# Input loads of a retention, mixer and MLP kernel: the second to fourth loads each wait for an earlier landing

## The reference

```python
# retention, per head h (8 heads of 64), token by token
state = gamma[h] * state + outer(k[t], v[t]);  x[t] = scale * q[t] @ state
# token mixer with angles
theta = x @ w_theta;  zr = x * cos(theta);  zi = x * sin(theta)
u = x + w_tok_r @ zr + w_tok_i @ zi
x2 = u + relu(u @ w_ch)
# token MLP, then channel MLP
u2 = x2 + (relu(x2.T @ w_tok1) @ w_tok2).T
out = u2 + relu(u2 @ w_ch1) @ w_ch2
```

## Time and profile before

| what | value |
|---|---|
| median of 3 runs | 435.96 us (435.9 to 437.29) |
| the profiled execution's own time | 435.77 us |
| its span in the trace | 434.0 us |
| TensorE busy | 426.8 us, 98% of the span |
| VectorE, ScalarE, GpSimd busy | 278.4, 158.3, 85.3 us |
| transfers, mean over the span | 97 GB/s |
| granted TensorE clock | 9 tenths or more in all 40 slices of the page |

### The profile page before, as it was taken

The page is one execution under the profiler, slowest core; times in us unless marked ns, Lnnn a source line. Parts: engine busy times, 40 slices in busy tenths (PEclk is TensorE's granted clock), DMA queues, the critical chain, the costliest instruction groups (busy, mean ns, idle before and its releaser), DMA issues.

```text
span 434.0 us, 6621 instructions
## 1 busy us (share of the span) xinstructions
PE 426.8 (98%) x2748; PEld 388.3 (89%) x2748; DVE 278.4 (64%) x383; ACT 158.3 (36%) x231; POOL 85.3 (20%) x75
## 2 busy tenths in 40 slices
PE   7999999999999999999999999999999999999997
PEld 4778878899999999999889988888888899999997
DVE  3799998799999995234415304525211599999951
ACT  1364564744455456112214311101202443555500
POOL 1322241000300006980005803303000110000000
PEclk9999999999999999999999999999999999999999
DMA  8975797540594102030000000003000468340121
GB/s 301 419 269 198 253 270 146 103 145 2 157 220 159 48 2 97 2 115 31 0 2 0 2 0 0 2 0 142 5 0 2 72 154 171 113 67 26 54 74 73
DMA packets 10478, 42.25 MB, mean 97 GB/s; under 512 B 1104, under 2 KB 3280, under 8 KB 8656
## 3 DMA queue, kind: packets, MB, share of 16 engines
q1 hardware_dynamic: 7344, 26.74, 16.6%
q0 software_dynamic: 2960, 14.94, 15.6%
q10 hardware_dynamic: 144, 0.14, 0.1%
HBM read 38.68 MB, written 3.15 MB: 96 GB/s over the span
## 4 chain that ended last, share of the span: by engine, by line
PE 96%; DVE 2%; DMA 1%; ACT 0%; issue 0%; ACTq 0%; DVEq 0%
PE ps L982 85%; PE ps L999 3%; PE ps L1039 3%; PE ps L1053 2%; PE ps L1130 1%; PE ps L1013 1%; PE ps L1029 1%; DMA qkv_in<-qkv 1%; DVE prob L712 1%; DVE h_ops_c L906 0%; DVE w_sq L696 0%; ACT h_ops_c L657 0%; DVE x_lo L736 0%; DVE res L731 0%; DVE res L942 0%
## 5 line engine op out<-in xcount | busy, mean ns | idle before, releaser
L982 PE MATMUL ps<-u,ch 128*128 128x512 f32 x432 | 98.1, 389 | 0.0
L982 PEld LDWEIGHTS ps<-u,ch 128*128 128x128 f32 x432 | 81.1, 188 | 16.8
L982 PE MATMUL ps<-tw,zs 128*128 128x384 f32 x504 | 88.1, 335 | 0.0
L982 PEld LDWEIGHTS ps<-tw,zs 128*128 128x128 f32 x504 | 87.3, 188 | 0.1
L982 PE MATMUL ps<-h_ops_c,w 128*128 128x384 f32 x312 | 57.0, 335 | 0.2
L982 PEld LDWEIGHTS ps<-h_ops_c,w 128*128 128x128 f32 x312 | 54.2, 188 | 0.8 <-DVE h_ops_c L906 0.8
L899 DVE SCALAR_TENSOR_TENSOR h_a<-ps,h_a 128x512 f32<-128x512 f32 (+1 forms) x16 | 8.9, 558 | 44.3 <-PE ps L982 26.3
L580 ACT ACTIVATE zs<-z 128x768 fp32r<-128x768 f32 x28 | 23.7, 846 | 37.0 <-PE ps L982 37.0
L982 PE MATMUL ps<-ut,w_sq 128*128 128x384 f32 x192 | 35.5, 338 | 0.0
L982 PEld LDWEIGHTS ps<-ut,w_sq 128*128 128x128 f32 x192 | 33.0, 188 | 0.0
L982 PE MATMUL ps<-w_sq,x_hi 128*128 128x512 f32 x96 | 30.7, 401 | 0.7 <-DVE w_sq L696 0.7
(11 more groups left out here) (106 smaller groups left out, 639.0 us busy)
## 6 DMA issues: line engine op xcount, KB each, us to landing
qkv_in<-qkv SPq DMA_DIRECT2D x11, 1024.0 KB, 7.5
raw<-tok POOLq DMA_DIRECT2D x7, 1152.0 KB, 9.0
stage<-weights SPq DMA_DIRECT2D x11, 512.0 KB, 3.4
w_raw<-ch POOLq DMA_DIRECT2D x7, 768.0 KB, 6.8
cols_out<-res SPq DMA_DIRECT2D x16, 192.0 KB, 1.8
raw<-tok SPq DMA_DIRECT2D x6, 384.0 KB, 8.6
w_raw<-ch SPq DMA_DIRECT2D x2, 768.0 KB, 5.3
raw<-tok POOLq DMA_DIRECT2D x3, 384.0 KB, 9.2
```

The source lines that it names most:

```text
L982: mm = pe.matmul(dst, left(l), right(r), start=first and n == 0, stop=last and n == 2, skip_group_check=True)
```

## The change

Four waits are put into SyncE's order of loads. The second chunk is issued when the first queries and keys have landed. The two halves of the angle weights are issued when the first group's second half has landed. The third chunk is issued when the second has landed. The first third of the token weights is issued when the second half of the angle weights has landed, and what follows it on SyncE (the fourth chunk and the rest) comes behind that wait. The order of the loads is the same, and no other engine's instructions differ.

```diff
             sp.dma_start(cst[:, C_OUT:N_CONST], consts[:, C_OUT:N_CONST]).then_inc(decay_in, 16)
+
+            sp.wait_ge(first_qk_in, 16)
             load_chunk(1)
+            sp.wait_ge(chunk_in[0], 16)
             for i in range(2):
                 at = slice(i * THETA_HALF, (i + 1) * THETA_HALF)
                 sp.dma_start(raw[:, 0, at], theta_w[:, at]).then_inc(theta_in[i], 16)
             for g in range(2, NG):
+                if g == 2:
+                    sp.wait_ge(chunk_in[1], 16)
                 load_chunk(g)
+                if g == 2:
+                    sp.wait_ge(theta_in[1], 16)
                 if g < 8:
                     load_third(g - 2)
```

## The result

The changed kernel takes 438.42 us (median of 6, 437.96 to 439.03) against 435.99 us for the kernel before timed beside it (6 executions, 435.9 to 437.46): +2.43 us. The ratio is 1.0049 with a 95% interval of 1.0033 to 1.0064, so the changed kernel is slower, by more than the 0.3% that the prediction took as the bound. The profiled execution has a span of 436.6 us against 434.0, +2.6.

What follows compares the result with a forecast made beforehand. TensorE was taken to bound the kernel from about 14 us, a chain of short steps before that. The only nonzero term, +0.8 us from later second-group scores, took 435.96 to 436.8 us; 8-in-10 range 435.8 to 438.3.

Steps and rivals of the forecast that it cites:

- likeliest case: Second chunk lands between 10.2 and 11.3, giving 436.8 us, own range 436.1 to 437.3; chance 57%.
- What bounds the kernel: TensorE from about 14 us on, a chain of short steps before; delay there reaches the end undiminished.
- The second chunk's landing: Issued at 5.6, taking 5.2 us, landing at 10.8; second group's scores start 0.8 us later.
- a long second chunk: Rival: second chunk takes 6.5 to 6.7 us, landing at 12.1 to 12.3; 438.1 to 438.3 us; chance 28%.
- The row of 20.93: Chunk in the profile before, issued at 20.93 with others still under way; it took 6.5 us.
- The 4.7: Time of the quicker of two chunks shown going into an idle queue, issued at 27.57; basis for taking 5.2 us.
- the row of 34.26: Chunk in the profile before, issued at 34.26 with nothing ahead of it; it took 6.7 us.
- Four waits, all from one place: The whole +0.8 us comes from the later start of the second group's scores; the other waits add 0.
- What the wait could give back: First queries and keys landing sooner: at most 0.3 us, ending at the second group's scores; worth 0.
- Angle weights, 0: First half lands at 12.0, `theta_high(0)` moves about 0.1 us; hidden with 0.7 us to spare, worth 0.
- Third chunk, 0: Issued at 10.9, landing about 0.9 us later at 15.9; hidden up to 1.36 us of lateness, worth 0.
- The price by the Trainium skill: Fit estimating 4.4 us for a chunk, landing at 10.0, sum +0.0; set aside for the trace's rows.

Runs made afterwards that it cites:

- The run with a pure delay: Kernel before, transfers untouched, with two products of zeros on TensorE ahead of the second group's scores: 439.21 against 435.82 us, ratio 1.0073.
- the repetition: The changed kernel, unaltered, timed once more on the chip of later runs: 438.98 against 436.04 us, ratio 1.005.
- the run behind the decay constants: Changed kernel with the second chunk waiting for the decay constants instead of the first queries and keys: 438.37 against 436.04 us, ratio 1.0046.
- the run with all four waits and TensorE kept busy: Changed kernel plus two products of zeros on TensorE between the first keys by values and second scores: 438.64 against 435.62 us, ratio 1.006.
- the run with 384 KB more: Changed kernel with a later 384 KB load of token weights moved ahead of the first wait: 439.61 against 436.04 us, ratio 1.0071.
- issue at 3.56: Changed kernel with the second chunk waiting for TensorE's first product of zeros: 435.98 against 436.04 us, ratio 0.9994.

## Why the prediction was right in its range and wrong in its likeliest case

The range went up to 438.3. The ratio of 1.0049 on the prediction's 435.96 gives 438.1; the median as it stands, 438.42, is 0.1 above that end. The likeliest case, 436.8, was too low by more than half the loss. That the range held is in part luck: in the profiled execution the chunk made 1.62 us, which alone would be 437.6, and 0.96 us came from two things that the sum had at nothing or not at all.

- **What bounds the kernel: right.** What was lost in the first 22 us was there at the end (+2.58, then +2.6). The run with a pure delay says the same, and that the price can be above one for one where VectorE and GpSimd collide.
- **The second chunk's landing: the mis-sized term.** "I take 5.2 us from issue to landing": it took 6.2 in the profiled execution, 7.0 in the repetition. The scores were later by 1.62 and 2.32 in place of 0.8. The rival "a long second chunk" had 6.5 to 6.7 and 438.1 to 438.3; its time came, and its landing lay between the two measured. It had 28% and should have had the larger part. The row of 20.93, issued with others still under way, was the one alike in kind. I weighed it less because it came late in the program; but the run behind the decay constants took 4.7 us at the start as well, from an empty stream, and the six profiles with the chunk issued at 5.3 to 5.7 have 5.8 to 7.2. The 4.7 was the row of another case. Nor was it sure there: the row of 34.26 took 6.7 with nothing ahead of it. And the transfers view of before has one more chunk, issued at 40.32, with one engine still at its share of the chunk before, which the prediction left out and which made it three of four above the 5.7 us where the long case begins:

```profile
qkv_in<-qkv SPq DMA_DIRECT2D x1, 1024.0 KB, 7.5
```

- **"Four waits, all from one place": right on the place.** The first wait alone costs +2.3; the other three alone +0.2, not told from none.
- **What the wait could give back, 0: right.** The first queries and keys came 0.1 us sooner, and that ended at the wait for the chunk.
- **Angle weights, 0: right.** `theta_high(0)` started at 12.92, 1.0 us later than before and 0.9 later than forecast, and its result still lay ready before VectorE came to it at 14.73.
- **Third chunk, 0: wrong.** It was issued at 11.64, not 10.9, took 6.7 us and came 3.4 us later than before, beyond the 1.36 I gave it. It took part in the sum, 0.46 us, and 0.9 in the repetition. It costs so only together with the first wait: with the wait for the second chunk kept and the first one gone, it was on time.
- **Not in the sum: the clock.** The idle time I forecast was followed by a stretch at 1.2 GHz that made 0.50 us. In the run with all four waits and TensorE kept busy the total was no lower, the third chunk being next; the changed kernel's own full-clock executions are some 0.6 us shorter, so how much the clock costs in the end stays open. The three terms of one execution don't add up independently: they are what was reached by each point.
- **The price by the Trainium skill** ("DMA: Bandwidth & Descriptors", section "Anatomy of one DMA — SWDGE (gpsimd) path"): its fit of 2.0 us plus the bytes over 436 GB/s gave 4.4 as an estimate. The fit is for transfers issued by GpSimd, and these are issued by SyncE. The quickest chunks here took 4.6 to 4.7; the second chunk, issued at 5.3 to 5.7, took 5.8 to 7.2.

What stays open: why a chunk issued at 5.3 comes so late and so unevenly. That about 2 us of work ahead is the reason is argued, not shown: with 2.9 us ahead, in the run with 384 KB more, it took 7.2 us, while the third chunk of the run without the first wait had 2.4 us ahead at 9.69 and took 5.2. Not tried: issues between 3.56 and 5.2 us, and chunks cut into smaller transfers.

## What to carry to other kernels

In this kernel a load that was issued early and waited in the queue behind others cost nothing, and holding it back until another had landed cost 2.4 us of 436 at the first loads of the program. Holding back was free where the stream had been full for some time (the other three waits) or where 3.7 us of transfers were still ahead (issue at 3.56). How much must be ahead is not settled. For the price of a late load take the row of the same kind (empty, ending or full stream), not the best one, and add what its idle time does to TensorE's clock and to the next load in turn. Where TensorE has a short gap near the start, try a small product of zeros in it: here it took away the executions of 437.4 us and left the others as they were.

## What the runs showed of the hardware

- At the start of the program a chunk of 1024 KB took 4.7 us into an empty stream (one profile) and 5.8 to 7.2 when issued at 5.3 to 5.7, with 2 to 3 us of transfers ahead (six profiles), so that an issue at 5.3 and one at 7.25 landed at much the same time (11.1 to 12.4, and 11.95). In the six, three or more of the 16 shares came late, in the changed kernel eight.
- Into an empty or nearly empty stream later in the program, six chunks of the kernel before and the changed one took 4.7 to 7.5 us. In all six 13 of the 16 shares were in by 4.8 us; what differs is when the last one came.
- Idle times of 1.4 to 2.0 us on TensorE, behind short bursts, were followed by some 3 us at 1.2 GHz in some executions (10 us in one) and not in others of the same kernel; with a product of half a microsecond or a whole one in the gap of 1.4 us none of 24 executions had a mean clock under 0.999.
- VectorE's `theta_low` and GpSimd's decayed keys, run at the same time, were 0.85 and 0.87 us longer than in the kernel before.
